# The opening of a fused DFT, gated MLP and routed-expert kernel: fewer filling products, three bank pairs, another order of splits and sums

## The chip, the cores and the metric

The kernel runs on one core of one Trainium2 chip. A core has five engines with queues of their own: TensorE (PE), VectorE (DVE), ScalarE (ACT), GpSimd (POOL) and SyncE (SP, which issues the transfers); they meet only at semaphores. The metric is the time of one launch on the device in microseconds. Of the kernel before, three runs gave 627.64, 627.88 and 629.44; the median is 627.88 us. The profiled execution took 628.87 us, of which its span (first to last instruction) is 626.7 us.

## The reference

```python
X = np.fft.fft(np.fft.fft(x, axis=1), axis=2).real       # x: 4 x 3072 x 256
x_prev = X shifted by one token, zero at the start of each sequence
xk = mu_k * X + (1 - mu_k) * x_prev ;  xr = mu_r * X + (1 - mu_r) * x_prev
k = np.maximum(xk @ w_k, 0)                              # 256 x 1024
v = k * k @ w_v                                          # 1024 x 256
y = sigmoid(xr @ w_r) * v                                # 12288 tokens of 256
# routing: 8 experts, 384 places each; a token goes to its argmax expert if a place is left
h = relu(disp @ w1) ; out = gate * (h @ w2)              # per expert 256x1024, 1024x256
```

Everything is fp32. Products of the large matrices are computed from a high part (rounded to the format fp32r) and a low part (what is left): high*high + high*low + low*high, three matmuls for one.

## The kernel before

A block called phase 1 computes, for four sequences of 3072 tokens, the 2-D DFT, the token mix, the MLP and the routing; phase 2 runs the eight experts. Channels lie on the partitions, tokens on the free axis.

**The DFT** has three steps. Its input x comes in five chunks of residues (`CHUNKS`: 3, 3, 3, 2, 1), each as an "own" and a "partner" half. `pair(seq, c)` on DVE adds the halves in place (L733; the last chunk has a small L731 first). **Step 1** (`step1`, PE L1008, L1010) multiplies chunk c into two PSUM banks, "far" then "near"; ACT copies far to SBUF (`far_out`), and DVE forms near + far and near - far (`step1_out`, L744, L745; for the last chunk a copy, L741). The banks are taken in rotation from `first_pairs` for sequence 0 (two pairs, h and r) and from `later_pairs` (one pair) for the others; a chunk waits until `step1_out` of the chunk that had its banks is done. **Step 2** (PE L1023) starts when all five `step1_out` are done and works in five groups of q (3, 3, 3, 3, 1): ACT evicts the odd bank (`odd_out`), DVE the even bank (`even_out`). **Step 3** (PE L1035) works in four groups of q, `GROUPS3`: 4, 4, 4, 1. ACT copies the odd bank (`copy_odd`), DVE writes sum and difference into the token-wide tile `xt` (`sums`, L761), and ACT mirrors columns within `xt` (`mirrors`, L578, an "outer" part that the first tile needs and an "inner" rest). One more small product gives channel 128 (`step3_edge`), which ACT evicts and two small transfers place into a row of `xt` (`place_edge`, SP L416, L418); DVE waits for them at `near_edge_in`.

**The opening** is this DFT for sequence 0, alone, since no other work is there yet (`first_dft` on each engine). PE issues products on zeros between the pieces (`keep_warm`, L365; one product is two matmul rows in the trace): 5 ahead of step 1, then 3, 1, 1, 0, 0 behind its chunks, and 3 behind step 3. Beside it the weights of the MLP are split: ACT rounds the high parts of `wk` in four pieces and of `wr` in one (L594, L596), POOL subtracts to get the low parts (L511, L513), then casts the high parts of `wv` in two halves (L516) and subtracts theirs (L519); ahead of these POOL waits for `consts_in` and copies three small tables for the routing (L506 to L508).

**The first token tile** starts with DVE's difference of neighbouring tokens (`difference`, L765, both inputs in SBUF), the mix (L772), ACT's rounding (L615), DVE's low part (L778). `first_ups` on PE (L1107, L1110; 12 matmuls) begins with the high part of half 0, goes on with its low part, and then half 1 the same way. Its first matmul also waits for `tables`, `wk_split`, `wr_split`. ACT evicts with `hidden` (relu, L632) after its last `high_part`, and from then on PE works tile by tile.

**Steady state.** Sequence s+1 is transformed while the six token tiles of sequence s run: tile numbers t = 0 to 5, of which `PAIRING` = 2 holds all five `pair` steps on DVE, `STEP1` = 3, `STEP2` = 4 and `STEP3` = 5 hold the DFT steps. Each engine's order within a tile is written out by hand in its `before(n)` and `after(n)`; nothing reorders it. x of the next sequence is loaded in tile 0. In tiles 2 to 5 of sequence 0 a piece of expert 0's weights is split as well (`up0_part`).

```python
first_pairs, later_pairs = [h_pair, r_pair], [r_pair]
first_quads, later_quads = [v_pair, r_pair, h_pair, v_pair], [r_pair, v_pair, r_pair, r_pair]
```

`first_quads` and `later_quads` name the bank pairs of the four groups of step 3.

## Time and profile before

| what | value |
|---|---|
| median of three runs | 627.88 us |
| profiled execution, its span | 628.87 us, 626.7 us |
| PE busy | 609.4 us (97%) |
| DVE busy | 447.9 us (71%) |
| ACT busy | 314.9 us (50%) |
| POOL busy | 110.1 us (18%) |
| PE's share of the chain that ended last | 91% |

Busy time counts an engine's instructions, without register and semaphore work. The chain that ended last is followed back from the last instruction, at each step to what released it. The granted clock of TensorE is 1.00 for full speed (2.4 GHz) and 0.50 for half (1.2 GHz). All times below count from the start of the span.

### The profile page before, as it was taken

The numbers are of one execution on the slowest core, as the hardware profiler recorded it, in microseconds if no ns is written. First come the engines' busy times: TensorE is split into PE (matmuls) and PEld (weight loads), VectorE is DVE, ScalarE is ACT, GpSimd is POOL, SyncE is SP. The second block draws the span as 40 slices with busy tenths as digits, with TensorE's granted clock in tenths as the row PEclk, the third lists the DMA queues.
The fourth block names the chain that finished last, engine by engine and source line by source line (L and its number), as shares of the span: only waits on it lengthen the run. The fifth ranks groups of instructions, "written<-read, shape, count | busy, mean of one in ns | idle before, by whom it ended". The sixth has DMA issues, their size and how long they took to land.

```text
span 626.7 us, 10475 instructions
## 1 busy us (share of the span) xinstructions
PE 609.4 (97%) x3388; PEld 522.9 (83%) x3388; DVE 447.9 (71%) x1017; ACT 314.9 (50%) x670; POOL 110.1 (18%) x105
## 2 busy tenths in 40 slices
PE   8979999999999999999999999999997999999995
PEld 4858888788888888888888888788886999999995
DVE  3587677977777687778886766787862777666671
ACT  1555455454545554545454446464543555654450
POOL 0530112020202011202020202030215111111111
PEclk9979999999999999999999999999998999999999
DMA  8419964251420033000000000060006634554100
GB/s 310 136 40 177 358 213 145 94 185 52 147 82 23 2 89 132 17 1 9 1 9 1 6 1 3 1 202 3 3 2 214 217 134 163 186 186 161 50 25 25
DMA packets 41006, 59.64 MB, mean 95 GB/s; under 512 B 4455, under 2 KB 31928, under 8 KB 40957
## 3 DMA queue, kind: packets, MB, share of 16 engines
q1 hardware_dynamic: 37116, 52.52, 26.7%
q0 software_dynamic: 3840, 6.52, 2.9%
q8 instruction: 23, 0.38, 0.3%
q14 instruction: 27, 0.21, 0.1%
HBM read 36.54 MB, written 26.91 MB: 101 GB/s over the span
## 4 chain that ended last, share of the span: by engine, by line
PE 91%; DVE 3%; issue 2%; ACT 1%; DMA 1%; POOL 0%; POOLq 0%; DVEq 0%; ACTq 0%
PE bank L289 73%; PE bank L1077 4%; PE bank L1023 3%; PE bank L1008 3%; PE bank L1035 2%; PE bank L365 2%; PE bank L1107 1%; PE bank L1416 1%; DVE xr_raw L765 1%; DMA got<-dispatched 1%; PE bank L1425 1%; PE bank L1110 1%; PE bank L1426 0%; PE bank L1429 0%; DVE square L873 0%
## 5 line engine op out<-in xcount | busy, mean ns | idle before, releaser
L289 PE MATMUL bank<-xk,wk 128*128 128x512 f32 x666 | 169.8, 398 | 0.3 <-ACT relu L632 0.3
L289 PE MATMUL bank<-k,wv 128*128 128x512 f32 x672 | 165.4, 396 | 0.0
L289 PEld LDWEIGHTS bank<-k,wv 128*128 128x128 f32 x672 | 125.6, 188 | 28.9
L289 PEld LDWEIGHTS bank<-xk,wk 128*128 128x128 f32 x666 | 123.2, 189 | 27.6 <-ACT relu L632 1.0
L632 ACT ACTIVATE relu<-bank 128x512 f32<-128x512 f32 x116 | 69.0, 598 | 123.9 <-PE bank L289 114.6
L529 POOL DMA_INDIRECT dispatched<-rows,slot x56 | 65.5, 1169 | 370.3 <-DVE slot L855 318.9
L873 DVE TENSOR_TENSOR square<-relu 128x512 f32<-128x512 f32 x116 | 79.9, 691 | 43.3 <-ACT relu L632 35.3
L868 DVE TENSOR_TENSOR k<-square,k 128x512 fp32r<-128x512 f32 x115 | 78.9, 686 | 2.8 <-ACT k L627 2.8
L627 ACT ACTIVATE k<-square 128x512 fp32r<-128x512 f32 x115 | 71.9, 625 | 8.3 <-DVE square L873 8.3
L289 PE MATMUL bank<-down_w,he 128*128 128x256 f32 x576 | 70.9, 284 | 0.0
L289 PEld LDWEIGHTS bank<-down_w,he 128*128 128x128 f32 x576 | 69.6, 192 | 0.0
L1329 ACT ACTIVATE he<-bank 128x384 fp32r<-128x384 f32 x64 | 31.5, 492 | 61.5 <-PE bank L1429 30.3
L1372 DVE SCALAR_TENSOR_TENSOR he<-bank,he 128x384 fp32r<-128x384 f32 x64 | 35.7, 558 | 37.0 <-ACT he L1329 34.1
L289 PE MATMUL bank<-xr,wr 128*128 128x512 f32 x180 | 47.3, 402 | 0.0
L1399 POOL DMA_INDIRECT out_rows<-ye,who x24 | 23.7, 988 | 116.5 <-DVE ye L1381 112.2
L289 PEld LDWEIGHTS bank<-xr,wr 128*128 128x128 f32 x180 | 32.8, 188 | 6.8
L887 DVE TENSOR_TENSOR x<-gate_r,bank 128x512 f32<-128x512 f32 x28 | 18.9, 686 | 21.3 <-PE bank L289 21.2
L615 ACT ACTIVATE xr<-xr_raw 128x512 fp32r<-128x512 f32 x30 | 18.9, 631 | 23.8 <-DVE xr_raw L772 23.4
L289 PE MATMUL bank<-xe,up 128*128 128x384 f32 x168 | 29.8, 334 | 0.0
L1077 PEld LDWEIGHTS bank<-fan,x 128*128 128x128 f32 x224 | 27.8, 190 | 2.0 <-DVE x L887 1.0
L289 PEld LDWEIGHTS bank<-xe,up 128*128 128x128 f32 x168 | 29.2, 188 | 0.0
L289 PE MATMUL bank<-xe,up_high 128*128 128x384 f32 x112 | 28.9, 338 | 0.0
(128 smaller groups left out, 720.2 us busy)
## 6 DMA issues: line engine op xcount, KB each, us to landing
out_rows<-blank SPq DMA_DIRECT2D x16, 768.0 KB
raw_up<-in_moe_w SPq DMA_DIRECT2D x8, 1024.0 KB, 23.5
raw_down<-in_moe_w SPq DMA_DIRECT2D x8, 1024.0 KB
x_area<-in_x SPq DMA_DIRECT2D x12, 384.0 KB, 3.8
y<-in_x SPq DMA_DIRECT2D x9, 384.0 KB, 5.0
dispatched<-blank SPq DMA_DIRECT2D x1, 3276.0 KB, 22.3
got<-dispatched SPq DMA_DIRECT2D x8, 409.5 KB, 3.2
first_partner<-in_x SPq DMA_DIRECT2D x3, 384.0 KB, 5.1
```

The lines of the kernel that those rows point to most:

```text
L289: done = nc.tensor.matmul(bank, w, x, start=first and i == 0, stop=last and i == len(terms) - 1)
L529: nc.gpsimd.indirect_dma_start(out=slots_dram, out_offset=bass.IndirectOffsetOnAxis(ap=slot[:, g:g + 1], axis=0), in_=rows[:, g, :], in_of ...
L615: nc.scalar.activation(high[:, 0, h, :], raw[:, h, :], ACT.Copy).then_inc(x_high, 1)
L627: nc.scalar.activation(k2_at(0, f), square[:, f % 2, :], ACT.Copy).then_inc(k2_high, 1)
L632: nc.scalar.activation(relu[:, f % 2, :], hb[f % 2][:, :], ACT.Relu).then_inc(hb_drained, 1)
L868: nc.vector.tensor_tensor(k2_at(1, f), square[:, f % 2, :], k2_at(0, f).bitcast(fp32), ALU.subtract).then_inc(squared, 1)
L873: nc.vector.tensor_tensor(square[:, f % 2, :], relu[:, f % 2, :], relu[:, f % 2, :], ALU.mult).then_inc(square_ready, 1)
L887: nc.vector.tensor_tensor(x3[:, h, :], gate_r[:, h, :], vb[h][:, :], ALU.mult).then_inc(x3_done, 1)
L1077: done = mm(tb[g][:, h * SPLIT:(h + 1) * SPLIT], x3[:, h, g * P:(g + 1) * P], fan[:, h, :], start=True, stop=True)
L1329: nc.scalar.activation(he[:, 0, f, :], hbe[f % 3][:, 0:cap], ACT.Relu).then_inc(he_high, 1)
L1372: nc.vector.scalar_tensor_tensor(he[:, 1, f, :], hbe[f % 3][:, 0:cap], 0.0, he[:, 0, f, :].bitcast(fp32), ALU.max, ALU.subtract).then_inc( ...
L1399: nc.gpsimd.indirect_dma_start(out=out, out_offset=bass.IndirectOffsetOnAxis(ap=who[:, i, j:j + 1], axis=0), in_=ye[:, i, j, :], in_offset ...
```

## The change

On PE the filling products of the opening become 4 ahead of step 1, then 1, 1, 0, 0, 0, and 4 behind step 3. Step 1 and 2 of sequence 0 rotate over three bank pairs instead of two, and step 3's groups of sequence 0 use v, h, r, v. On DVE `pair(0, 4)` comes ahead of `step1_out(0, ..., 2)`. ACT rounds a piece of `wk` behind each of the first four `odd_out` instead of the last four, and takes half of `wv`'s rounding over from POOL. POOL does `wk`, `wr`, one half cast of `wv`, then the subtraction in four quarters, and the three tables last. The waits for `tables` and `wr_split` move from PE's first product to where the data are used. Step 3's groups become 4, 4, 3, 2 for all sequences. The `pair` steps of the later sequences are spread over two tiles: chunks 0 and 1 in tile 1 (`PAIRING`), chunks 2, 3 and 4 in tile 2 (`PAIRING2`); `up0_part` stays in tiles 2 to 5.

```diff
-GROUPS3 = [(0, 4), (4, 8), (8, 12), (12, 13)]
+GROUPS3 = [(0, 4), (4, 8), (8, 11), (11, 13)]
...
-PAIRING, STEP1, STEP2, STEP3 = TILES - 4, TILES - 3, TILES - 2, TILES - 1
+PAIRING, PAIRING2, STEP1, STEP2, STEP3 = TILES - 5, TILES - 4, TILES - 3, TILES - 2, TILES - 1
...
+    WV_QUARTERS = [slice(k * FT // 4, (k + 1) * FT // 4) for k in range(4)]
...
-    first_pairs, later_pairs = [h_pair, r_pair], [r_pair]
-    first_quads, later_quads = [v_pair, r_pair, h_pair, v_pair], [r_pair, v_pair, r_pair, r_pair]
+    first_pairs, later_pairs = [h_pair, r_pair, v_pair], [r_pair]
+    first_quads, later_quads = [v_pair, h_pair, r_pair, v_pair], [r_pair, v_pair, r_pair, r_pair]
...
-                pool.wait_ge(consts_in, 16 * CONSTS)
-                nc.gpsimd.tensor_copy(earlier[:, :], small[:, 0:P])
-                nc.gpsimd.tensor_copy(ones[:, :], small[:, P:2 * P])
-                nc.gpsimd.tensor_copy(token[:, :], token0).then_inc(tables, 1)
                 for i, (h, cols) in enumerate(WK_PIECES):
                     pool.wait_ge(wk_high, i + 1)
                     nc.gpsimd.tensor_tensor(wk[:, 1, h, cols], raw_wk[:, h, cols], wk[:, 0, h, cols].bitcast(fp32), ALU.subtract).then_inc(wk_split, 1)
                 pool.wait_ge(wr_high, 1)
                 nc.gpsimd.tensor_tensor(wr[:, 1, :, :], raw_wr[:, :, :], wr[:, 0, :, :].bitcast(fp32), ALU.subtract).then_inc(wr_split, 1)
                 pool.wait_ge(wv_in, 16)
-                for half in WV_HALVES:
-                    nc.gpsimd.tensor_copy(wv[:, 0, half, :], raw_wv[:, half, :]).then_inc(wv_high, 1)
-                for k, half in enumerate(WV_HALVES):
-                    pool.wait_ge(wv_high, k + 1)
-                    nc.gpsimd.tensor_tensor(wv[:, 1, half, :], raw_wv[:, half, :], wv[:, 0, half, :].bitcast(fp32), ALU.subtract).then_inc(wv_split, 1)
+                nc.gpsimd.tensor_copy(wv[:, 0, WV_HALVES[1], :], raw_wv[:, WV_HALVES[1], :]).then_inc(wv_high, 1)
+                pool.wait_ge(wv_high, len(WV_HALVES))
+                for part in WV_QUARTERS:
+                    nc.gpsimd.tensor_tensor(wv[:, 1, part, :], raw_wv[:, part, :], wv[:, 0, part, :].bitcast(fp32), ALU.subtract).then_inc(wv_split, 1)
+                pool.wait_ge(consts_in, 16 * CONSTS)
+                nc.gpsimd.tensor_copy(earlier[:, :], small[:, 0:P])
+                nc.gpsimd.tensor_copy(ones[:, :], small[:, P:2 * P])
+                nc.gpsimd.tensor_copy(token[:, :], token0).then_inc(tables, 1)
...
-                        if i > 0:
-                            h, cols = WK_PIECES[i - 1]
+                        if i < len(WK_PIECES):
+                            h, cols = WK_PIECES[i]
                             act.wait_ge(wk_in, 16)
                             nc.scalar.activation(wk[:, 0, h, cols], raw_wk[:, h, cols], ACT.Copy).then_inc(wk_high, 1)
                     act.wait_ge(wr_in, 16)
                     nc.scalar.activation(wr[:, 0, :, :], raw_wr[:, :, :], ACT.Copy).then_inc(wr_high, 1)
+                    act.wait_ge(wv_in, 16)
+                    nc.scalar.activation(wv[:, 0, WV_HALVES[0], :], raw_wv[:, WV_HALVES[0], :], ACT.Copy).then_inc(wv_high, 1)
...
                     pair(0, 3)
+                    pair(0, 4)
                     step1_out(0, first_pairs, 2)
-                    pair(0, 4)
...
-                    if stage == PAIRING:
-                        pair(seq, 0)
+                    if stage == PAIRING2:
+                        pair(seq, 2)
                     elif stage == STEP1:
                         step1_out(seq, later_pairs, 0)
                     elif stage == STEP2:
@@ -919,7 +922,9 @@
                         sums(seq, later_quads, 1)
                     squares(n, 5)
                     if stage == PAIRING:
-                        pair(seq, 1)
+                        pair(seq, 0)
+                    elif stage == PAIRING2:
+                        pair(seq, 3)
                     elif stage == STEP1:
                         step1_out(seq, later_pairs, 1)
                     elif stage == STEP2:
@@ -933,7 +938,9 @@
                             difference(t + 1, h, n + 1)
                     squares(n, 6)
                     if stage == PAIRING:
-                        pair(seq, 2)
+                        pair(seq, 1)
+                    elif stage == PAIRING2:
+                        pair(seq, 4)
...
-                        keep_warm([3, 1, 1, 0, 0][c])
+                        keep_warm([1, 1, 0, 0, 0][c])
...
-                        last_use = [i for i in range(len(TRIPLES)) if first_pairs[i % 2] is first_quads[g]]
+                        last_use = [i for i in range(len(TRIPLES)) if first_pairs[i % len(first_pairs)] is first_quads[g]]
...
-                    keep_warm(3)
-                    pe.wait_ge(tables, 1)
+                    keep_warm(4)
                     pe.wait_ge(fan_in, 16 * 2 * DH)
                     pe.wait_ge(wk_split, len(WK_PIECES))
-                    pe.wait_ge(wr_split, 1)
                     pe.wait_ge(s3_summed, DH * QUADS)
...
+                    if m == 0:
+                        pe.wait_ge(tables, 1)
...
+                    if n == 0:
+                        pe.wait_ge(wr_split, 1)
...
-                keep_warm(5)
+                keep_warm(4)
```

DVE in step 1 of sequence 0, before (L733 is `pair`, L731 the small part of `pair(0, 4)`, L744 and L745 `step1_out`):

```order
L744 TENSOR_TENSOR y<-bank,far_copy 128x6x13x5
L745 TENSOR_TENSOR y<-bank,far_copy 128x6x13x5
L733 TENSOR_TENSOR x_area<-x_area,first_partner 128x512
L744 TENSOR_TENSOR y<-bank,far_copy 128x6x13x5
L745 TENSOR_TENSOR y<-bank,far_copy 128x6x13x5
L731 TENSOR_TENSOR apart<-x_area,first_partner 128x2
L733 TENSOR_TENSOR x_area<-x_area,first_partner 128x256
```

and in the change, where the same lines are L746, L747, L735 and L733:

```order
L746 TENSOR_TENSOR y<-bank,far_copy 128x6x13x5
L747 TENSOR_TENSOR y<-bank,far_copy 128x6x13x5
L735 TENSOR_TENSOR x_area<-x_area,first_partner 128x512
L733 TENSOR_TENSOR apart<-x_area,first_partner 128x2
L735 TENSOR_TENSOR x_area<-x_area,first_partner 128x256
L746 TENSOR_TENSOR y<-bank,far_copy 128x6x13x5
L747 TENSOR_TENSOR y<-bank,far_copy 128x6x13x5
```

Both sums of the last two chunks now stand together, ahead of the eviction of chunk 2.

PE in step 1 of sequence 0, before (L365 are the filling products, L1008 step 1; in brackets the semaphores):

```order
L1008 MATMUL bank<-c_first_sb,x_area 128x130 [waits x_paired,first_in_0]
L1008 MATMUL bank<-c_first_sb,x_area 128x130 x5
L365 MATMUL bank<-relu 128x512 x3
L1008 MATMUL bank<-c_first_sb,x_area 128x130 [waits x_paired,first_in_1]
L1008 MATMUL bank<-c_first_sb,x_area 128x130 x5
L365 MATMUL bank<-relu 128x512
L1008 MATMUL bank<-c_first_sb,x_area 128x130 [waits s1_drained,x_paired,first_in_2]
L1008 MATMUL bank<-c_first_sb,x_area 128x130 x5
L365 MATMUL bank<-relu 128x512
L1008 MATMUL bank<-c_first_sb,x_area 128x130 [waits s1_drained,x_paired,first_in_3]
```

and in the change (L366 and L1011):

```order
L1011 MATMUL bank<-c_first_sb,x_area 128x130 [waits x_paired,first_in_0]
L1011 MATMUL bank<-c_first_sb,x_area 128x130 x5
L366 MATMUL bank<-relu 128x512
L1011 MATMUL bank<-c_first_sb,x_area 128x130 [waits x_paired,first_in_1]
L1011 MATMUL bank<-c_first_sb,x_area 128x130 x5
L366 MATMUL bank<-relu 128x512
L1011 MATMUL bank<-c_first_sb,x_area 128x130 [waits x_paired,first_in_2]
L1011 MATMUL bank<-c_first_sb,x_area 128x130 x5
L1011 MATMUL bank<-c_first_sb,x_area 128x130 [waits s1_drained,x_paired,first_in_3]
L1011 MATMUL bank<-c_first_sb,x_area 128x130 x3
```

Three products are gone between the chunks, and chunk 2 no longer waits for a drained bank pair (`s1_drained`).

POOL's splits before its first scatter, before:

```order
L506 CAST earlier<-small 128x128 [waits consts_in]
L507 CAST ones<-small 128x128
L508 COPY token<-small 128x4
L511 ISA
L511 TENSOR_TENSOR wk<-raw_wk,wk 128x512 [waits wk_high] x4
L513 TENSOR_TENSOR wr<-raw_wr,wr 128x512 [waits wr_high]
L516 CAST wv<-raw_wv 128x1024 [waits wv_in]
L516 CAST wv<-raw_wv 128x1024
L519 TENSOR_TENSOR wv<-raw_wv,wv 128x1024 [waits wv_high] x2
```

and in the change:

```order
L508 ISA
L508 TENSOR_TENSOR wk<-raw_wk,wk 128x512 [waits wk_high] x4
L510 TENSOR_TENSOR wr<-raw_wr,wr 128x512 [waits wr_high]
L512 CAST wv<-raw_wv 128x1024 [waits wv_in]
L515 TENSOR_TENSOR wv<-raw_wv,wv 128x512 [waits wv_high]
L515 TENSOR_TENSOR wv<-raw_wv,wv 128x512 x3
L517 CAST earlier<-small 128x128 [waits consts_in]
L518 CAST ones<-small 128x128
L519 COPY token<-small 128x4
```

One cast has gone to ACT, the subtractions are half as long and twice as many, and the tables have moved behind them.

## Rows read from the trace of the kernel before

**Rows 1.** The page's part 1: busy time of each engine, share of the span, instructions.
```profile
PE 609.4 (97%) x3388; PEld 522.9 (83%) x3388; DVE 447.9 (71%) x1017; ACT 314.9 (50%) x670; POOL 110.1 (18%) x105
```

**Rows 2.** PE's waits, 44 to 470 us: line, waited for, us in total, times, longest.
```profile
PE bank L1077 <- DVE x L887: 0.4, 1, 0.4
PE bank L1035 <- DVE xt L761: 0.3, 2, 0.2
```

**Rows 3.** Chain of waits, 0 to 60 us: start us, us, what.
```profile
2.01 7.13 PE bank L365 x10
9.13 1.34 PE bank L1008 x12
10.47 2.58 PE bank L365 x6
...
19.62 0.30 DVE y L741
19.92 0.14 issue
20.06 5.96 PE bank L1023 x52
26.02 3.56 PE bank L1035 x32
...
32.72 0.66 DVE xt L761
...
34.22 2.91 DVE xr_raw L765
...
44.53 15.52 PE bank L289 x65
```

**Rows 4.** Timeline of DVE: start us, us, engine, line, operation [idle before <-releaser].
```profile
9.28 0.96 DVE L733 TENSOR_TENSOR x_area<-x_area,first_partner 128x768 f32<-128x768 f32 x1 [1.54 <-DMA first_partner<-in_x]
10.51 0.57 DVE L744 TENSOR_TENSOR y<-bank,far_copy 128x390 f32<-128x390 f32 x1 [0.28 <-PE bank L1008]
...
11.77 0.96 DVE L733 TENSOR_TENSOR x_area<-x_area,first_partner 128x768 f32<-128x768 f32 x1 [0.22 <-DMA first_partner<-in_x]
...
37.82 0.69 DVE L765 TENSOR_TENSOR xr_raw<-xt 128x512 f32<-128x512 f32 x1
...
93.81 1.39 DVE L887 TENSOR_TENSOR x<-gate_r,bank 128x512 f32<-128x512 f32 x2 [2.35 <-PE bank L289]
```

**Rows 5.** Timeline of POOL in the opening.
```profile
23.76 4.97 POOL L511 TENSOR_TENSOR wk<-raw_wk,wk 128x512 fp32r<-128x512 f32 x4
28.70 1.27 POOL L513 TENSOR_TENSOR wr<-raw_wr,wr 128x512 fp32r<-128x512 f32 x1
29.92 2.02 POOL L516 CAST wv<-raw_wv 128x1024 fp32r<-128x1024 f32 x2
31.90 4.66 POOL L519 TENSOR_TENSOR wv<-raw_wv,wv 128x1024 fp32r<-128x1024 f32 x2
```

**Rows 6.** Stretches: busy us of each engine, granted clock (PEclk), DMA share, GB/s.
```profile
35.20:37.90 2.70, 0.00 (x0) 0.00 (x0) 2.67 (x3) 0.00 (x0) 1.36 (x1) 1.00 0.00 1
38.80:41.30 2.50, 2.49 (x6) 2.02 (x7) 2.47 (x5) 1.83 (x6) 0.00 (x0) 0.50 0.00 0
```

**Rows 7.** Transfers issued 8 to 20 us: issue, count, KB, median us to landing.
```profile
c_second_sb<-in_c_second SPq DMA_DIRECT2D x1, 129.0 KB, 5.8
```

**Rows 8.** Timeline of SP's queue, the same columns as group 4.
```profile
9.26 0.45 SPq L424 DMA_DIRECT2D c_second_sb<-in_c_second  x1
...
34.90 0.62 SPq L418 DMA_DIRECT2D xt<-edge  x1
```

**Rows 9.** Timeline of ACT in the opening.
```profile
26.54 0.63 ACT L596 ACTIVATE wr<-raw_wr 128x512 fp32r<-128x512 f32 x1
...
39.98 0.63 ACT L615 ACTIVATE xk<-xk_raw 128x512 fp32r<-128x512 f32 x1 [0.67 <-DVE xk_raw L772]
...
42.09 0.62 ACT L615 ACTIVATE xr<-xr_raw 128x512 fp32r<-128x512 f32 x1
```

**Rows 10.** The same view near the end of phase 1.
```profile
475.50:477.30 1.80, 0.02 (x1) 0.03 (x1) 0.00 (x0) 0.00 (x0) 1.43 (x2) 1.00 0.77 236
...
478.40:481.60 3.20, 3.20 (x10) 3.20 (x11) 1.35 (x3) 0.96 (x3) 3.20 (x2) 0.50 1.01 363
```

More of the change, by code:

```diff
@@ L692, in after @@
                         mirrors(seq, 3)
-                    if seq == 1 and PAIRING <= n <= STEP3:
-                        up0_part(n - PAIRING)
+                    if seq == 1 and PAIRING2 <= n <= STEP3:
+                        up0_part(n - PAIRING2)
                     hidden(n, 7)
@@ L810, in first_dft @@
                     nc.vector.tensor_scalar(limit[:, :], expert_no, float(cap), float(cap), ALU.mult, ALU.add)
-                    dve.wait_ge(tables, 1)
                 def route_choose(m):
@@ L822, in route_choose @@
                     shifted = rows[:, :, P:SPLIT]
+                    if m == 0:
+                        dve.wait_ge(tables, 1)
                     dve.wait_ge(row_copied, CREDIT + GRP * (m + 1))
@@ L866, in low @@
                     if n == 0 and f == FT // 2:
-                        dve.wait_ge(wv_split, len(WV_HALVES))
+                        dve.wait_ge(wv_split, len(WV_QUARTERS))
                     nc.vector.tensor_tensor(k2_at(1, f), square[:, f % 2, :], k2_at(0, f).bitcast(fp32), ALU.subtract).then_inc(squared, 1)
@@ L947, in after @@
                     low(n, FT - 1)
-                    if stage == PAIRING:
-                        pair(seq, 3)
-                    elif stage == STEP2:
+                    if stage == STEP2:
                         even_out(seq, later_pairs, 3)
-                    if seq == 1 and PAIRING <= n <= STEP3:
-                        up0_part(n - PAIRING)
+                    if seq == 1 and PAIRING2 <= n <= STEP3:
+                        up0_part(n - PAIRING2)
                     if early:
@@ L962, in after @@
                         mix(t + 1, 3, n + 1)
-                        if stage == PAIRING:
-                            pair(seq, 4)
-                        elif stage == STEP1:
+                        if stage == STEP1:
                             step1_out(seq, later_pairs, 4)
@@ L1080, in route_counts @@
                 def route_counts(m):
+                    if m == 0:
+                        pe.wait_ge(tables, 1)
                     pe.wait_ge(onehot_ready, m + 1)
@@ L1126, in down @@
                         if n == 0:
-                            pe.wait_ge(wv_split, len(WV_HALVES))
+                            pe.wait_ge(wv_split, len(WV_QUARTERS))
                     for h in range(DH):
```

## The prediction

> **What bounds the kernel now.** I read the busy times first: PE works 97% of the span [rows 1], so a change can only pay where PE has pauses or does work that nobody needs. PE's waits show where the pauses are: between 44 and 470 us, nearly all of phase 1, there are two kinds, one of 0.4 us and two that make 0.3 us [rows 2]. What is left is the opening, and the chain of waits over the first 60 us is the view for it [rows 3]. The reader is to see three things there. First, PE's chain in step 1 is made of filling products as much as of work: 7.13 us ahead of it and 2.58 us behind chunk 0. Second, steps 2 and 3 (from 20.06 us) are PE work without a gap. Third, behind step 3 the chain leaves PE: DVE's sums end at 33.38 (32.72 + 0.66), and then one DVE instruction, the first difference, takes 2.91 us, where the same instruction takes 0.69 at 37.82 [rows 4]. POOL's two subtractions of `wv` run from 31.90 to 36.56 [rows 5], and the slow difference ends 0.57 us after them (37.13): it stood behind POOL's second one. PE had nothing to do meanwhile, its granted clock fell to half (1.2 GHz), and the first products of tile 0 ran at 0.50 [rows 6]. The first regular product starts at 44.53 [rows 3]. So the sum is: by how much does 44.53 move, plus the small pauses of [rows 2].
>
> **Step 1.** A filling product costs 2.58 / 3 = 0.86 us at full clock [rows 3]. One fewer ahead of step 1 moves chunk 0 from 9.13 to 8.27; it ends at 9.61. One filler, 10.47; chunk 1's sum is ready at 9.28 + 0.96 = 10.24 [rows 4], so it runs 10.47 to 11.81. One filler, 12.67. Chunk 2's sum ends at 11.77 + 0.96 = 12.73 [rows 4], and with a third bank pair nothing else holds the chunk: 12.8 to 14.1. From here DVE is the chain. It evicts chunk 1 from 12.73; an eviction is two instructions of 0.57, which overlap to 1.04 (10.51 to about 11.55) [rows 4], to 13.8. The sum of chunk 3 has two thirds of the columns, 0.65, to 14.4; that of chunk 4 with its small part 0.55, to 15.0. PE does chunk 3 by 15.4 and chunk 4 by 16.5. DVE evicts chunk 2 (1.04), chunk 3 (0.7) and chunk 4 (0.30 [rows 3]), to about 17.1, and with the 0.14 of issue step 2 starts at 17.3 instead of 20.06: 2.8 us. The unknown is when chunks 3 and 4 land. The transfer of `c_second` is issued behind them at 9.26 and lands 5.8 later, at 15.06 [rows 7, 8]. If they land at the latest just before it, the last sum ends at 15.6 and step 2 starts 0.6 later; if early, nothing changes. I take no delay, since chunks 0 to 2 landed 2.5 us apart, chunks 3 and 4 are two thirds and one third as large, and that puts them at 13.4 and 14.3.
>
> **Steps 2 and 3.** The same rows of PE, 5.96 + 3.56 and what follows, shifted by 2.8. Step 2 had no wait to lose, so its third pair is worth nothing. The last two groups of step 3 are 3 and 2 instead of 4 and 1. A q costs PE 3.56 / 8 = 0.45, so the sums of the third group may start 0.45 earlier; the DVE work of the two groups together is unchanged, the last mirrors are somewhat longer (0.1). I take 0.35. ACT has now a rounding of 1024 columns of `wv`, 2 x 0.63 = 1.26 us [rows 9], ahead of the first `copy_odd`. It delays the sums of group 0 by some 0.6; PE's next two groups (3.6 us) cover it. Without that cover it would cost 0.6. DVE can thus take the first difference at 34.22 - 2.8 - 0.35 = 31.1.
>
> **POOL.** The tables no longer stand in front. ACT's first piece of `wk` is done at 17.3 + 0.7 (odd bank) + 0.5 + 0.62 = 19.1; the pieces come one per group of step 2 (5.96 x 12 / 52 = 1.37), so the fourth subtraction runs 23.3 to 24.5 at 4.97 / 4 = 1.24 each [rows 5]. Then `wr` 1.27, one cast of 2.02 / 2 = 1.01, four quarters that together make 4.66 [rows 5]: to 31.5. Only the tables, 0.7, are behind it. DVE asks at 31.1, waits for the last quarter, and has the difference by 32.1 instead of 37.13: 5.0 us. If the tables go first too, 32.8.
>
> **What is late next.** Half 1's difference needs the edge row. SP issues the second edge transfer at 34.90 [rows 8], now 3.15 earlier, at 31.75. Its landing is bounded by rows only: not before its issue ends (0.62), and not after DVE used it at 37.82 without a wait, 2.92 after the issue. DVE itself is ready at 32.1 + 0.7 (mix) = 32.8. So the second difference starts between 32.8 and 34.7; I take 2.0 us for the landing, 33.75, nearer to the upper end. That is 4.1 ahead of 37.82: of the 5.0 won at POOL, 0.9 is given back to a transfer. From there difference, low part and mix (0.64 + 0.63 + 0.7) bring ACT's rounding of half 1 to 35.75, and from that rounding to the end of the last one ACT took 42.09 + 0.62 - 39.98 = 2.73 [rows 9], mirrors between them; to 38.5. PE at full clock would be done with the 12 products of `first_ups` at about 37.7, so ACT's order (relu comes behind the last rounding) is the end of this chain. Before, PE ended it at half clock. Relu 0.6 and PE's first regular product: 39.15 instead of 44.53, that is 5.4 us. What stood at half clock after 44.53 gives another 0.15.
>
> **Steady state.** The pause of 0.4 us at a tile's end in sequence 0 [rows 2] comes in the tile where DVE carries all five sums and a piece of expert 0; two sums (2 x 0.96) leave it, so it goes. Tile 1 takes them; DVE waits 2.35 us for PE there [rows 4], which covers 1.9. The pauses of 0.3 at step 3 wait for the sums of the third group, which are now a quarter smaller and start earlier. I take 0.6 of the 0.7. The waits moved on PE (`tables`, `wr_split`) are long met where they now stand: cost nothing.
>
> **Sum.** 5.4 + 0.15 + 0.6 = 6.15 us, made against the profiled execution: 628.87 - 6.15 = 622.7. That execution lies 1.0 above the median of the runs shown (627.88); taken off the median the forecast is 621.7.
>
> **Rivals.** *The clock falls all the same.* In the forecast PE ends its fillers behind step 3 at 32.8 and then works only some 2.6 us until 39.15, with pauses of 0.75, 0.6, 0.9 and 1.5 us. For it: near the end of phase 1 PE had an idle stretch of 1.8 us and stood at 0.50 soon after [rows 10]. Against it: the idle stretch of the opening was 2.7 us and more [rows 6], and no single pause is as long now. Price: `first_ups` ends at 38.95 instead of 37.7 (0.45 past ACT), and the regular products run at half speed until the clock is back, which costs half of 2 to 5 us. Together 1.5 to 3, so 623.2 to 624.7, middle 624. The Trainium skill (TensorE: Matmul & The Clock Gate, Part 1) says that the default is the slow clock and that idleness brings it back; by that alone the short pauses would be harmless and the forecast stands, but the row with 1.8 us idle makes me keep the rival.
>
> *POOL is still in the way.* If its queue runs 0.5 to 1.2 us later than I have it, DVE's difference and mix, all with both inputs in SBUF, each meet another quarter. Difference, mix and second difference then come 0.7 late: 622.4. In the one case the trace shows, at 34.22, POOL's next instruction went first. The Trainium skill (SBUF — State Buffer, section on SBUF's two sides) says that a VectorE instruction with two SBUF inputs and a GpSimd one that reads SBUF exclude each other for a whole instruction; the 2.91 us agree. By that rule the three table copies hold DVE as well, which is the 32.8 above.
>
> *Tile 1 is too full.* If the added sums cost more than the 2.35 of slack, or x has not landed, each of three tiles 1 loses about 0.5: 623.2.
>
> *Slower: the clock falls in step 1.* Fewer fillers and a pause of about 0.8 us ahead of step 2. If TensorE stood at half clock through steps 2 and 3, their 12 us of full-speed work would take 24: 621.7 + 12 = 633.7. It decides once more than 6.15 us of that work runs at half clock. Against it: PE is busy some nine tenths of 8.3 to 16.5 us, and no pause there is over 1 us.
>
> **Chances.** Forecast 0.50; clock falls 0.33; POOL 0.08; tile 1 0.05; slower 0.03; the rest for what I don't see. The likeliest gives 621.7. Its low end: the edge lands early and all bounds fall well, 1.2 less, and some 0.6 for the spread of the runs, 619.9. Its high end joins the clock rival, 625.1. A difference under 0.3% (1.9 us) can't be told from none; all cases but the last gain more, save a clock that stays low for long, so faster 0.94, same 0.03, slower 0.03.
>
> **What would show it.** Step 2's first product at 17.3 (later by 0.6: the landing); PE's step 1 rows with 20 filling rows in all; the first difference at about 0.6 to 1.1 us instead of 2.91, started near 31; DVE idle before the second difference, ended by the edge transfer; granted clock 1.00 all the way from 32 to 45; the first regular product near 39.15; no wait of PE at the end of tile 2. The prediction is wrong if the second difference does not wait, if the clock shows 0.50 anywhere ahead of 45 us, or if PE waits in tile 1.

## The result and the profile after

| | median us | lowest to highest | runs |
|---|---|---|---|
| kernel before | 627.68 | 627.18 to 629.44 | 6 |
| the change | 622.01 | 621.08 to 622.92 | 6 |

The ratio is 0.9906, 95% interval 0.9891 to 0.9921: faster by 0.9%, 5.67 us in the medians. The forecast was 621.7, range 619.9 to 625.1. The profiled execution of the change took 621.71 us, span 619.6, against 628.87 and 626.7 of before.

The busy times first, which answer to [rows 1]. PE has 4.3 us less to do (fewer fillers, less at half clock), so that some 2.8 of the 7.1 us are idle time that went.

```profile
PE 605.1 (98%) x3382; PEld 519.1 (84%) x3382; DVE 447.7 (72%) x1019; ACT 315.5 (51%) x671; POOL 110.1 (18%) x106
```

The timeline of PE in the opening (start us, us, engine, line, operation, in brackets idle time before and who ended it); this answers to the chain in [rows 3].

```profile
2.00 5.87 PE L366 MATMUL bank<-relu 128*128 128x512 f32 x8 [2.00 <-DVE relu L719]
7.96 1.58 PE L1011 MATMUL bank<-c_first_sb,x_area 128*128 128x130 f32 x12
...
10.48 1.58 PE L1011 MATMUL bank<-c_first_sb,x_area 128*128 128x130 f32 x12
11.90 1.02 PE L366 MATMUL bank<-relu 128*128 128x512 f32 x2
12.98 3.01 PE L1011 MATMUL bank<-c_first_sb,x_area 128*128 128x130 f32 x22
...
17.39 5.96 PE L1026 MATMUL bank<-c_second_sb,y 128*120 128x129 f32 x52 [0.57 <-DVE y L743]
...
29.72 3.60 PE L366 MATMUL bank<-relu 128*128 128x512 f32 x8
34.17 1.18 PE L1110 MATMUL bank<-xk,wk 128*128 128x512 f32 x4 [0.84 <-ACT xk L617]
35.19 0.62 PE L1113 MATMUL bank<-xk,wk 128*128 128x512 f32 x2
36.19 1.20 PE L1110 MATMUL bank<-xk,wk 128*128 128x512 f32 x4 [0.38 <-ACT xk L617]
37.22 0.63 PE L1113 MATMUL bank<-xk,wk 128*128 128x512 f32 x2
38.76 3.06 PE L290 MATMUL bank<-xk,wk 128*128 128x512 f32 x12 [0.90 <-ACT relu L634]
```

The reader is to see that the first regular product stands at 38.76 instead of 44.53, and that its last wait is for ACT's relu. From here on this start is called the *first regular product*; it is the yardstick of the experiments, since an opening ends there. It carries the landing of x with it: over the nine profiles that have the change's step 1 (this one and eight of the experiments), step 2 starts anywhere from 17.16 to 17.88. The distance from step 2's start to the first regular product repeats better: 21.37 us in the change, 21.37 in a second profile of it (m), and 21.35 or 21.36 in d, f, h and i, whose edits don't touch what lies between. So a few tenths are read from that distance.

POOL's timeline, against [rows 5]:

```profile
19.42 5.23 POOL L508 TENSOR_TENSOR wk<-raw_wk,wk 128x512 fp32r<-128x512 f32 x4 [18.15 <-ACT wk L594]
...
25.83 1.03 POOL L512 CAST wv<-raw_wv 128x1024 fp32r<-128x1024 f32 x1
26.94 4.98 POOL L515 TENSOR_TENSOR wv<-raw_wv,wv 128x512 fp32r<-128x512 f32 x4
31.86 0.75 POOL L517 CAST earlier<-small 128x128 bf16<-128x128 f32 x1
32.56 0.84 POOL L518 CAST ones<-small 128x128 bf16<-128x128 f32 x1
```

and DVE's, where L767 is the difference that took 2.91 us at L765 before, with a wait ahead of the second one that [rows 4] does not have:

```profile
31.17 1.29 DVE L767 TENSOR_TENSOR xr_raw<-xt 128x512 f32<-128x512 f32 x1 [0.50 <-ACT xt L578]
32.50 0.75 DVE L774 SCALAR_TENSOR_TENSOR xk_raw<-xr_raw,mu_k,xt 128x512 f32<-128x512 f32 x1
33.52 0.69 DVE L767 TENSOR_TENSOR xr_raw<-xt 128x512 f32<-128x512 f32 x1 [0.26 <-DMA xt<-edge]
```

That wait is for the edge row, issued by SP at 31.86. ACT's end of the chain, against [rows 9]:

```profile
35.50 0.63 ACT L617 ACTIVATE xk<-xk_raw 128x512 fp32r<-128x512 f32 x1 [0.84 <-DVE xk_raw L774]
...
37.60 0.62 ACT L617 ACTIVATE xr<-xr_raw 128x512 fp32r<-128x512 f32 x1
38.12 1.06 ACT L634 ACTIVATE relu<-bank 128x512 f32<-128x512 f32 x2
```

Three stretches of the change (busy time of PE, PEld, DVE, ACT, POOL, then granted clock, DMA share, GB/s). Beside [rows 6], the first two show 1.00: `first_ups` with its pauses, and the regular products behind it. The third, beside [rows 10], is the turn to phase 2.

```profile
33.30:38.80 5.50, 3.37 (x14) 2.15 (x13) 5.12 (x8) 4.66 (x12) 0.24 (x2) 1.00 0.01 3
38.76:44.50 5.74, 5.74 (x25) 4.68 (x26) 4.82 (x10) 3.90 (x7) 0.00 (x0) 1.00 0.74 184
...
467.30:470.40 3.10, 3.10 (x6) 1.65 (x5) 0.00 (x0) 0.33 (x2) 0.00 (x0) 0.50 0.61 155
```

Last the waits of PE between the first regular product and the end of phase 1, against [rows 2]:

```profile
PE bank L290 <- ACT relu L634: 0.9, 1, 0.9
PE bank L1038 <- DVE xt L763: 0.5, 2, 0.3
```

**Where the time went.** I follow one small product, the first routing product of each tile (PE L1084 before, L1087 after), through phase 1, of which the trace holds 14 tiles: the walk over the tiles ends once every expert's places are taken. It is 5.91 us earlier in tile 1 (72.47, now 66.56), 6.53 in tile 3 (127.45, now 120.92), and 6.37 at the end (464.19, now 457.82): the opening, plus 0.6 for the pause that left tile 2, minus 0.1 in each of the two tiles with step 3. So 6.37 of the 7.1 us of the profiled executions come from where the prediction looked. The remaining 0.7 lies at the turn between the phases: the first product of phase 2's second round (PE L1416 before, L1421 after) stands at 488.31 and 481.19, which is 7.1 apart. The clock fell there in both: before, its 3 us at 0.50 covered expert 0's first products (478.4 to 481.6, [rows 10]); in the change they lie at 467.3 to 470.4, mostly under filling products. The medians differ by 5.67, less than either; no run here separates how much of the 6.37 an unprofiled execution loses again. The clock may have a part in it, which isn't shown: the granted clock, averaged over an execution, was 0.990 in the profiled one of before, and lay between 0.990 and 0.996 over 17 executions of before beside a to d; in the six of the change it was 0.994 to 0.998.

### The profile page after: what moved, and what is told of

Same layout as the page of the kernel before. It is cut to its first block and busy times, and to the rows that moved or that the text cites. A ratio compares the mean times of both kernels' runs of the same rounds, so it can differ in the third digit from the quotient of the medians.

```text
span 619.6 us, 10469 instructions
## 1 busy us (share of the span) xinstructions
PE 605.1 (98%) x3382; PEld 519.1 (84%) x3382; DVE 447.7 (72%) x1019; ACT 315.5 (51%) x671; POOL 110.1 (18%) x106
## 5 line engine op out<-in xcount | busy, mean ns | idle before, releaser
L1334 ACT ACTIVATE he<-bank 128x384 fp32r<-128x384 f32 x64 | 31.5, 492 | 60.3 <-PE bank L290 29.6
```

The lines of the kernel that those rows point to most:

```text
L1334: nc.scalar.activation(he[:, 0, f, :], hbe[f % 3][:, 0:cap], ACT.Relu).then_inc(he_high, 1)
```

## The experiments

All are edits of the change, except b, which edits the kernel before. Three groups ran, each on one chip with its own runs of before: a to d (before 627.84), e to h (627.89), and i, j, l, m (627.33). The edits of a, b, j and h are shown in short, partly in words.

**a: without the splits.** POOL's and ACT's splits in their old form and order, all else as changed: step 1, the groups of step 3 and the spread sums stay.

```diff
+pool.wait_ge(consts_in, 16 * CONSTS)          # three table copies first
 wk (4 pieces), wr
-one half cast; wait for both; four quarters; tables
+two half casts; two halves, each behind its cast
```

> The change with the weight splits in the old order: POOL does its three tables first, then wk, wr, both casts of wv and the subtraction in two halves, ACT rounds the last four pieces' places as before and nothing of wv. Step 1's edits stay. Theory 1 (POOL's queue set the old opening, and step 1 alone only makes PE and DVE wait longer for it): POOL still waits for the constants at 23 us and ends at 36.6, the first difference ends at 37.1, the clock falls, the first regular product is at 44.5 as in the kernel before; only the pause in tile 2 stays won, so about 627.0 us. Theory 2 (the gain is mostly step 1's 2.7 us, handed on): first regular product about 41.5 to 42, 624.5 us.

Measured: 628.89 (10 runs, 627.37 to 630.06), ratio 1.0012 [0.9999, 1.0025]. Step 2 starts at 17.88, over 2 us earlier than before, and the first regular product at 44.90 stands 0.4 later than before. The time lies 1.9 above the 627.0 that was expected. POOL and DVE of this run:

```profile
25.11 0.29 POOL L507 CAST earlier<-small 128x128 bf16<-128x128 f32 x1 [23.84 <-DMA mu_r<-in_moe_mu_r]
...
34.90 5.55 POOL L520 TENSOR_TENSOR wv<-raw_wv,wv 128x1024 fp32r<-128x1024 f32 x2
```

```profile
35.39 2.84 DVE L779 TENSOR_TENSOR xk<-xk_raw,xk 128x512 fp32r<-128x512 f32 x1
38.16 2.83 DVE L773 SCALAR_TENSOR_TENSOR xk_raw<-xr_raw,mu_k,xt 128x512 f32<-128x512 f32 x1
```

POOL starts only when the last constant has landed, at 25.1, whatever PE did; its two halves then end at 40.5. In the kernel before they had landed by 23.05; the landing of the last constant varies between the profiles, 23.0 to 25.1, and this one is the latest. So up to 2 us of the 44.90 can be the landing, and the size of the loss in this one profile isn't a price. DVE comes earlier into POOL's queue, so that not one instruction stands behind a half but two, and the granted clock falls to 0.50 from 39 us on. That nothing is gained rests on the ten runs: all of step 1's 2.2 us were given back, and by itself that part of the change is worth nothing.

**b: the splits alone.** The kernel before with only the new splits and moved waits.

```diff
-tables; wk; wr; two casts; two halves         # POOL
+wk; wr; one cast; four quarters; tables
+ACT: wk pieces one group earlier, one half cast of wv
```

> The kernel before with nothing but the new splits: POOL wk, wr, one cast, four quarters, tables last, ACT one wk piece earlier and half of wv, the waits for tables and wr_split at their use. Theory 1: POOL ends about 34.5 (31.9 plus the 2.7 us by which step 2 is later), the first difference ends at 35.2, the second starts when the edge lands, 34.9 + 1.66 = 36.6, and the first regular product comes at 38.8 + (36.6 - 33.5) = 41.8: 2.7 us gained by itself, about 625.0 us. Theory 2 (the splits matter little): under 1 us gained, first regular product later than 43.5. If both theories of cost were simply additive the two parts a and b would make up the whole 5.8; theory 1 says that a gives about 0 and b half, and that the rest exists only with both.

Measured: 625.18 (8 runs, 624.83 to 626.57), ratio 0.9958 [0.9947, 0.9969]. The first regular product is at 41.26, 3.3 earlier than before. The difference meets little of POOL's work, and behind it stands the edge row:

```profile
33.66 0.93 DVE L767 TENSOR_TENSOR xr_raw<-xt 128x512 f32<-128x512 f32 x1 [0.47 <-ACT xt L578]
34.62 0.75 DVE L774 SCALAR_TENSOR_TENSOR xk_raw<-xr_raw,mu_k,xt 128x512 f32<-128x512 f32 x1
36.01 0.69 DVE L767 TENSOR_TENSOR xr_raw<-xt 128x512 f32<-128x512 f32 x1 [0.63 <-DMA xt<-edge]
```

The two parts do not add up: nothing, 2.7 us, and 5.7 together. Once POOL is out of the way, every microsecond of step 1 reaches the first product: b's step 2 starts at 19.50, 2.1 later than the change's, and from there it takes 21.76, as g does (21.75), which has b's groups. The granted clock stays at 1.00 here from 33.3 to 41.3, although PE idles for 1.72 us ahead of `first_ups`.

**j: only the tables first.** Quarters and ACT's cast stay; the three copies, with their wait for the constants, go back to the front.

```diff
+pool.wait_ge(consts_in, 16 * CONSTS)
+copies of earlier, ones, token
 wk pieces ...
```

> The change with POOL's three small tables in front of the splits again, and nothing else undone. Theory 1 (what stood in the way was the wait for the constants, which land at 23 to 25 us): POOL begins wk at 24 to 26 instead of 19.4, its last quarter ends at 35.5 to 37.5, DVE's difference, mix and low parts each wait for a piece of it, first regular product 41.5 to 43.5, some 3 to 4.5 us lost. Rival (the cast that ACT took over was the larger part): under 1.5 us lost.

Measured: 627.31 (one run), first regular product at 42.98, 4.2 later than the change. POOL, DVE and PE:

```profile
23.90 0.29 POOL L507 CAST earlier<-small 128x128 bf16<-128x128 f32 x1 [22.63 <-DMA mu_r<-in_moe_mu_r]
...
31.89 6.63 POOL L519 TENSOR_TENSOR wv<-raw_wv,wv 128x512 fp32r<-128x512 f32 x4
```

```profile
32.40 1.64 DVE L774 SCALAR_TENSOR_TENSOR xk_raw<-xr_raw,mu_k,xt 128x512 f32<-128x512 f32 x1
...
37.31 1.76 DVE L774 SCALAR_TENSOR_TENSOR xk_raw<-xr_raw,mu_k,xt 128x512 f32<-128x512 f32 x1
```

```profile
39.79 2.07 PE L1110 MATMUL bank<-xk,wk 128*128 128x512 f32 x4 [1.13 <-ACT xk L617]
```

This is the clearest picture of the two engines. Four DVE instructions of 0.69 to 0.75 each take 1.64 to 1.76, and POOL's four quarters take 6.63 instead of 4.98: they go in turn, one of DVE, one of POOL. The starts show it: POOL's at 31.89, 33.45 and 35.13, DVE's at 32.40, 33.96 and 35.64, each half a microsecond behind; what an instruction waits for the other engine is counted in its time. PE then pauses 1.13 ahead of the products of half 1, which run at half pace (2.07 for four instead of 1.18; the granted clock is 0.50 from about 36.5 to 43). The place of three copies of 0.2 to 0.3 us is the largest single part of the change, because of what they wait for. The Trainium skill (SBUF — State Buffer, SBUF: two separate sides) says that the pair shared by VectorE and GpSimd is locked for a whole instruction by whoever starts first; the trace agrees, and shows besides that the lock passes to and fro between two full queues.

**i: halves for quarters.** POOL subtracts `wv` in two halves again.

```diff
-                for part in WV_QUARTERS:
+                for part in WV_HALVES:
```

> The change with POOL's subtraction of wv in two halves instead of four quarters; ACT's share and the tables' place stay. In the change DVE asks for its first difference at 31.2 while the last quarter runs to 31.9. Theory 1 (POOL's queue ends at the same time either way, the size of its pieces decides nothing here): the first difference is done at 32.3 to 32.5, the second still waits for the edge, first regular product within 0.1 of 38.8. Rival (short pieces are what let DVE in): the first difference ends later than 33.0 and the first regular product comes 0.5 or more later.

Measured: 622.59 (one run), first regular product at 38.79, the first difference 1.03. The two halves take 4.70 where the four quarters take 4.98, so the difference is done at 32.25, 0.2 earlier; but the second one then waits 0.52 for the edge row instead of 0.26. The size of the pieces decides nothing once DVE asks at their end.

**c: two bank pairs.**

```diff
-    first_pairs, later_pairs = [h_pair, r_pair, v_pair], [r_pair]
+    first_pairs, later_pairs = [h_pair, r_pair], [r_pair]
```

(and the old order of step 3's pairs)

> The change with two bank pairs in the opening (h and r) instead of three; step 3 of sequence 0 takes v, r, h, v again. Theory 1 (chunk 2 is bound by its landing, the third pair only frees chunk 4): chunk 4 waits for the eviction of chunk 2 (ends 16.4) and runs 16.4 to 17.5, step 2 starts at 18.0 instead of 17.4, step 2 and 3 have no gap, first regular product 0.3 to 0.6 later. Rival (the third pair is what let chunk 2 start early): chunk 2 starts later than 13.3, step 2 later than 18.5.

Measured: 624.75 (one run); the first regular product 41.52, 2.8 later than the change, where a few tenths were expected. PE, then the clock:

```profile
16.72 0.46 PE L1011 MATMUL bank<-c_first_sb,x_area 128*128 128x130 f32 x2 [0.89 <-DVE y L747]
...
18.49 7.62 PE L1026 MATMUL bank<-c_second_sb,y 128*120 128x129 f32 x52 [0.48 <-DVE y L743]
```

```profile
19.20:22.20 3.00, 3.00 (x16) 3.00 (x15) 0.63 (x2) 1.01 (x2) 1.26 (x1) 0.50 1.04 284
```

Step 2 starts 1.1 us later (18.49 instead of 17.39), of which some 0.2 is x, since chunk 2 starts at 13.16 instead of 12.98; and then step 2 itself takes 7.62 instead of 5.96, since the clock stood at 0.50 for its first part, with PE busy throughout. Both make the 2.8. This is the "slower" rival of the prediction, small: PE had been idle for 0.89 us ahead of chunk 4 and for 0.48 ahead of step 2, and the clock fell half a microsecond into step 2. In b and d, with a single pause of 0.48 us ahead of step 2, it took 5.96. But the fall was seen in one execution, and the pauses alone don't explain it: in b the clock stayed up through one of 1.72. That two pairs bring the clock down, and the third keeps it up, is a guess; the wait of about 0.9 is what c shows, and the 1.66 is what a fall here costs.

**d: the fillers as before** (5 ahead; 3, 1, 1 between).

```diff
-                        keep_warm([1, 1, 0, 0, 0][c])
+                        keep_warm([3, 1, 1, 0, 0][c])
...
-                keep_warm(4)
+                keep_warm(5)
```

> The change with the filling products of the kernel before ahead of and in step 1 (5, then 3, 1, 1). Theory 1 (PE's fillers, not the landings, set the old step 1): chunk 0 at 9.1, chunk 1 at 13.0, step 2 between 19.0 and 19.9, everything behind it shifted by that, first regular product 40.5 to 41.3. Rival (DVE and the landings set it): step 2 before 18.0 and first regular product before 39.5.

Measured: 625.05 (one run); chunk 1 starts at 12.56, step 2 at 19.55, the first regular product at 40.91. The four more products are some 3.4 us of work at 0.86 each; 2.2 us of it push step 2 back, and these 2.2 go straight into the end.

**f: no fillers in step 1 at all.**

```diff
-                        keep_warm([1, 1, 0, 0, 0][c])
...
-                keep_warm(4)
```

> The change without any filling product ahead of or within step 1 (the four behind step 3 stay). It asks what the remaining fillers of step 1 buy. Theory 1: TensorE begins step 1 at half clock, a chunk takes 2.7 instead of 1.34 us, chunks 1 to 4 follow each other with hardly a gap and step 2 starts 1.5 to 3.5 us later, partly at half clock itself; first regular product 40.3 to 42.3, 623.5 to 625.5 us. Rival (landings and DVE set step 1 anyway): step 2 starts before 18.0, no difference in time.

Measured: 622.72 (4 runs, 621.31 to 623.18), ratio 0.9908 [0.9884, 0.9932]; first regular product 38.68. PE:

```profile
7.52 4.99 PE L1011 MATMUL bank<-c_first_sb,x_area 128*128 128x130 f32 x24 [7.52 <-DVE x_area L735]
12.90 3.02 PE L1011 MATMUL bank<-c_first_sb,x_area 128*128 128x130 f32 x22 [0.39 <-DVE x_area L735]
```

The first two chunks take 4.99 instead of twice 1.58, and it costs nothing: they are through at 12.51, ahead of chunk 2's sum, which PE waits for until 12.90, and by then the pace is full. The view's clock doesn't tell of the slow start:

```profile
7.50:12.50 5.00, 4.98 (x24) 4.59 (x24) 2.69 (x4) 0.99 (x2) 0.00 (x0) 1.00 1.03 393
```

It shows 1.00 where most of the products run at half pace, so in the first 12 us of a profile the pace is to be read from the products and not from the clock's column. My expectation of a loss of 1.5 to 3.5 us was wrong. The fillers that the change left in step 1 buy nothing.

**e: no fillers behind step 3.**

```diff
-                    keep_warm(4)
```

> The change without the four filling products behind step 3. This prices the clock. Theory 1: PE is idle from 29.9 to 34.2, the granted clock falls to 0.50 ahead of first_ups, whose 12 products then take twice as long; they end at 39.5 to 40 instead of 37.9 and are again what relu waits for; the regular products run at half clock for a few us more. First regular product 40.3 to 40.8, in all 3 to 4 us slower than the change, 625 to 626. Rival (the chain of DVE, the edge and ACT hides the clock): first regular product before 39.5 and under 1 us lost.

Measured: 622.77 (4 runs, 622.01 to 623.64), ratio 0.9916 [0.9893, 0.9939]; first regular product 39.42, 0.66 later. Step 2 started 0.23 earlier here (17.16), so the distance between the two is 22.26 instead of 21.37, 0.9 more. PE and the clock:

```profile
33.94 2.04 PE L1109 MATMUL bank<-xk,wk 128*128 128x512 f32 x4 [4.29 <-ACT xk L617]
...
39.42 3.06 PE L290 MATMUL bank<-xk,wk 128*128 128x512 f32 x12 [0.45 <-ACT relu L634]
```

```profile
34.00:38.30 4.30, 4.30 (x10) 3.38 (x11) 4.15 (x7) 3.14 (x9) 0.00 (x0) 0.50 0.00 0
```

The clock did fall, for nearly all of `first_ups`, and cost 0.9 us where 3 to 4 were expected. PE at half pace keeps relu waiting for only 0.8 us behind ACT's last rounding, which it did not delay; and the granted clock was back at 1.00 at about 38.3, ahead of the regular products. So the four products behind step 3 go with a clock that stays up, as the change wants, and in this profile that is worth about 0.9. The medians (622.77 and 622.01, on two chips) can't tell so little from none.

**g: groups 4, 4, 4, 1.**

```diff
-GROUPS3 = [(0, 4), (4, 8), (8, 11), (11, 13)]
+GROUPS3 = [(0, 4), (4, 8), (8, 12), (12, 13)]
```

> The change with step 3's groups 4, 4, 4, 1 again, for all sequences. The trace of the change has PE waits of 0.5 us in two tiles with step 3 where the kernel before had 0.3. Theory 1 (the split gains in the opening and loses in the tiles): the first difference and everything behind it 0.3 to 0.4 later unless the edge hides it, the two tiles with step 3 0.1 shorter each (36.2 instead of 36.3 us from one routing product to the next), in all the same time within 0.3. Rival (the split does nothing in the opening since POOL and the edge are later): first regular product within 0.1 of 38.8.

Measured: 623.26 (one run). The first regular product is 0.42 later (39.18), since the first difference starts at 31.59 instead of 31.17 (0.38 once step 2's start is taken off). The tiles with step 3 take 36.22 and 36.25 instead of 36.31 and 36.32, and PE's waits there are the old ones:

```profile
PE bank L1038 <- DVE xt L763: 0.3, 2, 0.2
```

The new groups help the opening and cost 0.1 us in each of the two tiles with step 3.

**h: all five sums in tile 2.**

```diff
-        if stage == PAIRING: pair(seq, 0), pair(seq, 1)      # tile 1
-        elif stage == PAIRING2: pair(seq, 2 .. 4)            # tile 2
+        if stage == PAIRING2: pair(seq, 0 .. 4)
```

> The change with the five pair steps of a later sequence again all in tile 2. Theory 1: the stretch of PE between the routing products of tiles 1 and 2 of sequence 0 takes 27.8 instead of 27.2 us, 0.6 us, and nothing in tiles 2 of the other sequences, which carry no piece of expert 0. Rival (the pause went for another reason, the earlier opening): 27.2 as in the change.

Measured: 623.81 (one run). The step from tile 2's routing product to the next takes 27.81 instead of 27.18, and the wait of [rows 2] is back:

```profile
PE bank L1078 <- DVE x L890: 0.4, 1, 0.4
```

**l and m: a next version, and the change again beside it.** Three edits: groups 4, 4, 3, 2 for sequence 0 alone; DVE mixes half 1 ahead of the low parts; ACT takes its first relu ahead of the last rounding.

```diff
+LATER3 = [(0, 4), (4, 8), (8, 12), (12, 13)]              # sequences 1 to 3
...
                     difference(0, 1, 0)
-                    low_part(0, 0)
                     mix(0, 1, 0)
-                    mix(0, 2, 0)
+                    low_part(0, 0)
                     low_part(1, 0)
+                    mix(0, 2, 0)
...
+                    hidden(0, 0)
+                    high_part(3, 0)
```

> The change with three things more. Step 3's groups are 4, 4, 3, 2 only for sequence 0 and 4, 4, 4, 1 for the others (the tiles with step 3 were 0.1 us longer with the new groups). Behind the second difference DVE does the mix of half 1 ahead of the low parts, so that ACT rounds it at about 34.9 instead of 35.5. ACT evicts the first product of tile 0 ahead of its last rounding. Theory 1 (behind the edge the order of DVE and ACT is what is late): first_ups ends at 37.2 instead of 37.9, first regular product 38.1 to 38.3 instead of 38.8, 0.2 more in the tiles, in all 0.6 to 0.9 faster than the change. Rival (PE waits for the low part of half 0 instead, or the later order comes back as a wait at the gate product): within 0.3 of the change.

> The change itself, beside the kernel of the run l_next on the same chip, so that the two can be compared run by run: 621.1 to 622.9 us as before, first regular product at 38.4 to 38.9.

Measured: l 621.89 (6 runs, 620.75 to 622.81), ratio 0.9913 [0.9897, 0.9929]; m 622.64 (6 runs, 621.53 to 623.28), 0.9926 [0.9911, 0.994]. In the medians l is 0.75 faster; the intervals overlap, so it isn't shown. In l's profile x came 0.4 later (step 2 at 17.72, against 17.36 in m), and still the first regular product was 0.16 earlier (38.73 in m); from step 2's start it takes 20.85 instead of 21.37, 0.5 less:

```profile
35.97 0.73 PE L1122 MATMUL bank<-xk,wk 128*128 128x512 f32 x2 [0.27 <-DVE xk L789]
...
38.57 1.67 PE L291 MATMUL bank<-xk,wk 128*128 128x512 f32 x6 [0.47 <-ACT relu L643]
```

PE now waits 0.27 for the low part of half 0, as the rival had it, but that wait isn't the one that ends last.

What the first regular product says of each part, beside the change's 38.76 and its 21.37 from step 2's start:

| taken back | first regular product | later by | from step 2's start |
|---|---|---|---|
| all splits (a) | 44.90 | 6.1 | 27.02 |
| place of the tables (j) | 42.98 | 4.2 | 25.37 |
| third pair (c), with the clock's fall | 41.52 | 2.8 | 23.03 |
| fewer fillers in step 1 (d) | 40.91 | 2.2 | 21.36 |
| fillers behind step 3 (e) | 39.42 | 0.7 | 22.26 |
| groups 4, 4, 3, 2 (g) | 39.18 | 0.4 | 21.75 |
| quarters (i) | 38.79 | 0.0 | 21.35 |

Even without a, which holds j and i, they sum to far more than the 5.8 that were won, since a single part taken back stops the others from paying.

## Why the prediction was right

**Step 1** was forecast at 8.27, 10.47, 12.8 for chunks 0 to 2 and 17.3 for step 2; it came at 7.96, 10.48, 12.98 and 17.39. The term "no delay" for chunk 4's landing was wrong, and luck covered it: I had 14.3, and DVE waited until 14.81.

```profile
14.81 0.16 DVE L733 TENSOR_TENSOR apart<-x_area,first_partner 128x2 f32<-128x2 f32 x1 [0.43 <-DMA first_partner<-in_x]
...
16.96 0.28 DVE L743 COPY y<-bank 128x130 f32<-128x130 f32 x1
```

From there DVE has no gap until step 2 can start, so up to 0.4 us of this wait is in step 2's start. The forecast came within 0.1 all the same, because DVE took 1.8 us from the end of chunk 4's sum (15.43) to the end of the last copy (17.24), where I had 2.1.

**Steps 2 and 3** were forecast to let DVE ask at 31.1; it asked at 31.17. Taking the groups back (g) cost 0.4 there, 0.35 forecast.

**POOL** was forecast to be through at 31.5 and was at 31.92, its subtractions of `wv` taking 4.98 instead of the 4.66 that I had taken from [rows 5]: I had priced four quarters as two halves, and halves again take 4.70 in i. The difference was done at 32.46 (forecast 32.1). The rival "POOL is still in the way" would have shown two DVE instructions stretched; one was, by 0.6. The tables behind took 0.75 and 0.84 instead of 0.29: now POOL waits for DVE, and nobody for POOL.

**The edge row** is the term I had only bounds for. With 2.0 us from issue to landing the second difference was to start at 33.75; it started at 33.52, 1.66 after SP's issue at 31.86. Its wait is there (0.26), and again in b (0.63), so the transfer is what is late next, as forecast.

**ACT and the end.** Last rounding of half 1 at 35.50 (35.75), `first_ups` done at 37.85 (37.7), first regular product at 38.76 (39.15): 5.77 us instead of 5.4. Of the 0.4 more, 0.25 is the edge row. The stretch from that rounding to the end of the last one, mirrors between them, was as forecast (2.72, 2.73). The other 0.14 is behind it: relu begins 0.1 before the last rounding ends. What stood at half clock behind 44.53 gave 0.14, as the 0.15 forecast (5.77 at the first regular product, 5.91 in tile 1).

**Steady state.** The pause of tile 2 went, 0.61 us, and h brings it back. The pauses at step 3 were forecast to shrink by 0.2 to 0.3 in all; this step failed. They grew, to 0.5 from 0.3 [rows 2], and the two tiles lost 0.1 each. The mistake was to look at when the sums could start and not at what stands ahead of them on DVE, and at when PE asks:

```profile
202.24 0.69 DVE L871 TENSOR_TENSOR k<-square,k 128x512 fp32r<-128x512 f32 x1
202.84 0.97 DVE L763 TENSOR_TENSOR xt<-bank,odd_copy 128x360 f32<-128x360 f32 x2
```

The sums of the third group stand behind a square of tile work and start only 0.1 earlier than before, counted from the tile's routing product. PE, with a quarter less to do in the third group, asks for the bank 0.45 earlier; the shorter sums are done 0.35 earlier, so PE waits 0.1 longer at 203.96.

**The sum** was 6.15 against 6.37 at the end of phase 1: 0.37 too little for the opening, 0.2 too little for tile 2, some 0.4 too much for step 3. The forecast from the median, 621.7, missed by 0.3, within the 1.8 us by which six runs scatter. That closeness is partly luck: between the profiled executions the sum was 1.0 too small (7.16, of which 0.7 fell at the turn of the phases, where it had no term), and between the medians it was 0.5 too large (5.67).

**The clock rival**, at 0.33, did not come in the profile: 1.00 in all stretches of the opening. (In the first 12 us the view shows 1.00 too, where f has it beside half pace; the sign "0.50 anywhere ahead of 45 us" can be read only from there on.) Experiment e made it come, and its price was wrong: 0.9, not 1.5 to 3. The part for `first_ups` was about right, 0.45 forecast and relu waiting 0.8 for PE. The part for the regular products, 1 to 2.5, was nothing, since the clock was back 1.1 us ahead of them. **The slower rival**, at 0.03, deserved more thought: c shows its mechanism at 1.66 us, and why the clock fell there stays open. I had looked only at the sum of PE's busy time and the longest pause. The Trainium skill (TensorE: Matmul & The Clock Gate, Part 1) has idleness bring the slow clock back, and e agrees (PE idle from 29.7, 0.50 from 31.5); the pauses that went ahead of the fall in c were under 1 us each, with PE busy between them, while b kept 1.00 through 1.72, so the length of the pauses alone does not tell the two apart.

## What to carry to other kernels

When one engine's chain is shortened, ask first which other engine's queue the next step meets, and whether that queue starts with a wait for something late: three short copies behind a late transfer cost more to put back than any other single part here. Two edits that each free one of two parallel chains must be judged together, since one alone may measure as nothing. And when a group boundary is moved inside a steady loop, compare what stands ahead of the work on the engine that does it, not the length of the group.

## What the hardware showed that I had not expected

- VectorE and GpSimd, both with SBUF operands and full queues, took turns instruction by instruction in j: 1.64 to 1.76 us for each DVE instruction of 0.7, and 6.63 us for four POOL ones that take 4.98 alone. DVE's sums with one input in PSUM were not stretched beside the same POOL work: two of 360 columns took 0.97 at 29.03, amid POOL's quarters, and 0.97 at 202.84, with POOL idle.
- TensorE's granted clock fell to 0.50 in c after idle pauses of 0.89 and 0.48 us, with products between them, while in the change it stayed at 1.00 through pauses of 0.84, 0.38 and 0.90 between 33.3 and 38.8, and in b through one of 1.72.
- The clock's column shows 1.00 in the first microseconds of the span, where f's first products run at half pace (24 rows in 4.99 us). The same four filling products at the start took 5.33 us in c, 5.87 in the change and 6.46 in e.
- Some 6.8 us at half clock (about 31.5 to 38.3; PE idle for the first 2.4) cost 0.9 us in e, where ACT's chain ran beside; in step 2 of c, where PE alone binds, 3.4 us at half clock cost 1.66.
- The small transfer that fills the edge row took 1.66 us from its issue to the instruction that waited for it, in the change and in b alike.
- The last constant landed between 23.0 and 25.1 us in the fourteen profiles, and POOL's old order waits for it: 23.05 before, 23.90 in j, 25.11 in a.
